# Two feed-forward layers on one core: 96 in place of 128 weight columns in one of five output products

## The chip, the cores and the metric

The kernel runs on one core of one Trainium2 chip. A core has five engines that run side by side and meet at semaphores: TensorE (PE, the matrix multiplier, whose weight loads the profile lists apart as PEld), VectorE (DVE), ScalarE (ACT), GpSimd (POOL) and SyncE (SP, which here only issues DMAs). The metric is the time of one execution on the device in microseconds; the median of several runs counts.

## The reference, cut to what matters

A softmax-weighted causal convolution of seven taps over 8192 tokens of 192 features, then two feed-forward layers:

```python
gate = 1.0 / (1.0 + np.exp(-(x @ w_gate)))        # x (8192, 192), w_gate and w_val (192, 1536)
y = gate * (x @ w_val) @ w_out                    # w_out (1536, 192)
h = y @ w_in                                      # w_in (192, 2048)
g = np.where(h > 0.0, h, np.exp(np.minimum(h, 0.0)) - 1.0)
z = g @ w_out2                                    # w_out2 (2048, 192)
```

Everything is float32.

## The kernel before

Features and hidden units lie on the partitions, tokens along the free axis. The tokens are cut into 16 blocks of T = 512. For each block there is a G phase (the gated layer: 12 tiles of 128 hidden units) and an E phase (the second layer: 16 tiles of 128, taken in 8 pairs).

Each float32 operand of a matmul is split into a high part and a low part (what the rounding of the high part left over), both of type fp32r. A product is then made of high by high, low by high and high by low. Low by low is not wanted: it is smaller than the rest by the square of the rounding.

TensorE works in two halves. A matmul on `rows` LOW (partitions 0 to 63) and one on UP (64 to 127) run side by side, each with its own weights of 64 rows by 128 columns, and each streams the 512 tokens. The code interleaves the two: in the loop over `s`, one LOW and one UP matmul are issued in turn. I call such a pair of places a slot. A G step (one tile) has 14 slots: 9 for the hidden units (`hid_mm`, HID = 9) and 5 for a tile's share of the outputs (`product`). LOW takes its 9 hidden matmuls first and the 5 products after, UP the 5 products first. An E step (a pair of tiles) has 19 slots, 9 and 10.

The 192 outputs of a layer lie in two banks. `acc[0]` (`y_acc_a`, `z_acc_a`) holds the first 128 outputs. `acc[1]` (`y_acc_b`, `z_acc_b`) holds the last 64 twice over: its lower 64 partitions sum the products with the high part of the weights, its upper 64 those with the low part, and the two halves are added later (ACT's `take_y_b` or `take_z`, then DVE). The weights for this lie side by side in 128 columns that begin at `both_b`: 64 high columns, then 64 low columns. The five kinds of `product` are:

- 0: high part of the hidden tile by the high weights of the first 128 outputs
- 1: low part of the hidden tile by the same weights
- 2: high part by the low weights of the first 128 outputs
- 3: high part by the 128 columns at `both_b`
- 4: low part by the 128 columns at `both_b`

So in kind 4 the first 64 columns give a wanted sum (low by high), and the last 64 give low by low. A matmul of kind 4 also carries semaphore increments: `share_done` on LOW, `up_b_done` on UP at the end of a step's products.

The last four tiles of the whole run have no partner. Their 20 products run after the last slot on all 128 rows at once. Over the run there are 5100 slots with two matmuls and 20 with one, 10220 matmuls in all, each with a weight load of its own.

Around this ACT bends (`curve`) and makes the high parts, DVE multiplies, makes the low parts and sums the taps, SP issues the loads of weights and tokens and the stores.

Of the kernel before, what the change touches and what calls it, by code (L numbers as in the profile page):

```python
# [12 lines left out]
P = 128  # L13
# [3 lines left out]
MAIN = 3 * P + OUT  # L17
LOW = slice(0, HALF)
UP = slice(HALF, P)
HID = 9  # L20
RING = 4
RAW_G_SLOTS = 8
# [11 lines left out]
def ffn_kernel(nc, conv_w, x_windows, g_weights, e_weights, out):  # L34
# [16 lines left out]
    with ExitStack() as ctx:  # L51
# [114 lines left out]
        def _(sp):  # L166
# [15 lines left out]
            def swap_x(j):  # L182
                sp.wait_ge(x_ready, 2 * j + 1)
                sp.dma_start(xs[LOW, 4:6].bitcast(F32), xs[UP, 0:2].bitcast(F32)).then_inc(x_swapped, 16)
                sp.dma_start(xs[UP, 4:6].bitcast(F32), xs[LOW, 0:2].bitcast(F32)).then_inc(x_swapped, 16)

            def swap_y(n, inp=ys):
                sp.wait_ge(y_free, 2 * n + 1)
                sp.dma_start(inp[LOW, 4:6].bitcast(F32), inp[UP, 0:2].bitcast(F32)).then_inc(y_swapped, 16)
                sp.dma_start(inp[UP, 4:6].bitcast(F32), inp[LOW, 0:2].bitcast(F32)).then_inc(y_swapped, 16)  # L190

# [39 lines left out]
        def _(pe):  # L231
            def hid_mm(rows, acc, w, inp, s, last=HID - 1):


                part, kind = divmod(s, 3)
                at = P * part + (MAIN + HALF if kind == 2 else 0)
                features = (0, 4, 2)[part] + (1 if kind == 1 else 0)
                return nc.tensor.matmul(acc[:], w[rows, at:at + P], inp[rows, features],  # L238
                                        start=s == 0, stop=s == last)
# [6 lines left out]
            def e_tile_share(t, base, acc):  # L246
                at, lo_a = (3 * P, 3 * P + MAIN + HALF) if t % 2 == 0 else (2 * MAIN, 2 * MAIN + 2 * P)
                return Share(acc, ew[:, t // 2], at, at + P, lo_a, t % RING, base + t + 1,
                             t == 0, t == NE - 1)

            def product(rows, share, kind, start, stop):


                at = (share.hi_a, share.hi_a, share.lo_a, share.both_b, share.both_b)[kind]
                part = (0, 1, 0, 0, 1)[kind]
                return nc.tensor.matmul(share.acc[kind // 3][:], share.w[rows, at:at + P],  # L256
                                        h_split[rows, share.slot, part], start=start, stop=stop)

            def share_and_kind(shares, k):


                tiles = len(shares)
                if k < 2 * tiles:
                    return shares[k // 2], 2 * (k % 2)
                if k < 3 * tiles:
                    return shares[k - 2 * tiles], 1
                return shares[(k - 3 * tiles) // 2], 3 + (k - 3 * tiles) % 2
# [4 lines left out]
            def up_share_waits(shares, k, step):  # L272
                share, kind = share_and_kind(shares, k)
                if kind == 0:
                    pe.wait_ge(hi_done, share.done)
                if kind == 1:
                    pe.wait_ge(lo_done, share.done)
                if k == 0:
                    wait(pe, low_a_done, step - LAG)
                if k == 3 * len(shares):  # L280
                    wait(pe, share_done, shares[0].done - 1)

            def low_share_waits(shares, k, step):
                if k == 0:
                    pe.wait_ge(up_a_done, step - LAG + 1)
                if k == 3 * len(shares):
                    pe.wait_ge(up_b_done, step - LAG + 1)

            def up_share(shares, k):
                share, kind = share_and_kind(shares, k)  # L290
                mm = product(UP, share, kind, share.first and kind in (0, 3), False)
                if k == 3 * len(shares) - 1:
                    mm.then_inc(up_a_done, 1)
                if k == 5 * len(shares) - 1:
                    mm.then_inc(up_b_done, 1)

            def low_share(shares, k):
                share, kind = share_and_kind(shares, k)
                mm = product(LOW, share, kind, False, share.last and kind in (1, 4))
                if k == 3 * len(shares) - 1:  # L300
                    mm.then_inc(low_a_done, 1)
                if kind == 4:
                    mm.then_inc(share_done, 1)

            def opening(inp):


                def both(t, part, kind):
# [3 lines left out]
                    lower = hid_mm(LOW, gate, gw[:, t], inp, s, last)  # L312
                    upper = hid_mm(UP, val, gw[:, t], inp, s, last)
                    if s == last:
# [32 lines left out]
            def g_phase(base, step, n, prev, inp=xs, acc=y_acc):  # L347
# [9 lines left out]
                for t in range(0 if prev else 3, NG):  # L357
# [18 lines left out]
                    count = 5 * len(shares)  # L376
                    for s in range(HID + count):
                        if s < count:
                            up_share_waits(shares, s, step + t)
                        if s >= HID:  # L380
                            low_share_waits(shares, s - HID, step + t)
                        if s == count and prev == "E" and t < 2:
                            pe.wait_ge(hidden_done, base - 2 + 2 * t)
                        if s < HID:
                            mm = hid_mm(LOW, gate, gw[:, t], inp, s)
                            if s == HID - 1:
                                mm.then_inc(hid_done, 1)
# [61 lines left out]
            for t in range(NE - 4, NE - 1):  # L449
                share = e_tile_share(t, end + NE, y_acc)  # L450
                pe.wait_ge(hi_done, share.done)
                product(slice(0, P), share, 0, False, False)
                product(slice(0, P), share, 2, False, False)
                product(slice(0, P), share, 3, False, False)
                pe.wait_ge(lo_done, share.done)
                product(slice(0, P), share, 1, False, False)
                product(slice(0, P), share, 4, False, False).then_inc(share_done, 1)
            share = e_tile_share(NE - 1, end + NE, y_acc)
# [445 lines left out]
```

## Time and profile before

| | us |
|---|---|
| median of 3 runs | 1187.38 (1187.08 to 1187.71) |
| the profiled execution, its time | 1185.75 |
| the profiled execution, its span | 1184.0 |
| TensorE matmul busy in the span | 1166.5 (99%) |
| TensorE weight load busy | 1058.8 (89%) |
| VectorE busy | 925.2 (78%) |
| ScalarE busy | 629.8 (53%) |
| GpSimd busy | 89.6 (8%) |

The page of the profile gives each engine's busy time, then the span in 40 slices, the DMA queues, the chain of work that ended last, and the costliest groups of instructions. Matmuls are pipelined and their ends are modelled. The start times in the timeline are therefore the ones to read, and a duration of 386 ns for a matmul doesn't mean that the next one starts 386 ns later. The span begins with the first instruction; the run's time is 1.75 us longer than it. The granted TensorE clock over the span is 1.000 of full speed.

### The profile page before, as it was taken

The numbers are of one execution on the slowest core, as the hardware profiler recorded it, in microseconds if no ns is written. First come the engines' busy times: TensorE is split into PE (matmuls) and PEld (weight loads), VectorE is DVE, ScalarE is ACT, GpSimd is POOL, SyncE is SP. The second block draws the span as 40 slices with busy tenths as digits, with TensorE's granted clock in tenths as the row PEclk, the third lists the DMA queues.
The fourth block names the chain that finished last, engine by engine and source line by source line (L and its number), as shares of the span: only waits on it lengthen the run. The fifth ranks groups of instructions, "written<-read, shape, count | busy, mean of one in ns | idle before, by whom it ended". The sixth has DMA issues, their size and how long they took to land.

```text
span 1184.0 us, 27136 instructions
## 1 busy us (share of the span) xinstructions
PE 1166.5 (99%) x10220; PEld 1058.8 (89%) x10220; DVE 925.2 (78%) x1497; ACT 629.8 (53%) x1093; POOL 89.6 (8%) x87
## 2 busy tenths in 40 slices
PE   5999999999999999999999999999999999999998
PEld 4988889998888888888888899999999889999998
DVE  7888777787777877778777787777777777787786
ACT  6556545465554555545455464554646545465554
POOL 4371001010010100101000010100101001010000
PEclk9999999999999999999999999999999999999999
DMA  6021101001010010100101001110101101001000
GB/s 209 20 72 37 32 18 35 31 18 31 18 35 31 18 31 18 42 25 18 31 18 49 18 18 31 36 31 18 24 24 36 31 18 35 31 18 31 10 11 27
DMA packets 14022, 38.04 MB, mean 32 GB/s; under 512 B 2224, under 2 KB 2224, under 8 KB 14000
## 3 DMA queue, kind: packets, MB, share of 16 engines
q1 hardware_dynamic: 13776, 37.60, 10.9%
q8 instruction: 15, 0.25, 0.1%
q10 hardware_dynamic: 224, 0.14, 0.1%
q14 instruction: 7, 0.06, 0.0%
HBM read 15.71 MB, written 6.29 MB: 19 GB/s over the span
## 4 chain that ended last, share of the span: by engine, by line
PE 97%; POOL 1%; DVE 1%; DMA 1%; ACT 0%; issue 0%; SPq 0%; DVEq 0%
PE hid L238 54%; PE z_acc_a L256 15%; PE y_acc_a L256 11%; PE z_acc_b L256 9%; PE y_acc_b L256 7%; POOL gw L815 1%; DMA raw_g<-g_weights 1%; DVE mixed L648 0%; POOL gw L823 0%; PE y_acc_a L238 0%; DVE ys L655 0%; SPq L175 0%; PE y_acc_b L238 0%; ACT ys L606 0%; DVE z_out L702 0%
## 5 line engine op out<-in xcount | busy, mean ns | idle before, releaser
L238 PE MATMUL hid<-xs,gw 64*128 64x512 f32 x3240 | 606.0, 386 | 0.0
L238 PEld LDWEIGHTS hid<-xs,gw 64*128 64x128 f32 x3240 | 501.7, 184 | 35.6 <-DVE h_split L675 0.6
L238 PE MATMUL hid<-ys,ew 64*128 64x512 f32 x2160 | 478.5, 387 | 0.0
L489 ACT CAST h_split<-hidden 128x512 fp32r<-128x512 f32 x448 | 277.0, 618 | 273.2 <-DVE hidden L717 231.4
L484 ACT ACTIVATE curve<-hid 128x512 f32<-128x512 f32 x446 | 263.3, 597 | 262.5 <-PE hid L238 262.3
L238 PEld LDWEIGHTS hid<-ys,ew 64*128 64x128 f32 x2160 | 376.2, 184 | 25.4 <-DVE h_split L675 0.8
L256 PE MATMUL z_acc_a<-h_split,ew 64*128 64x512 f32 x1440 | 365.4, 387 | 0.0
L675 DVE TENSOR_TENSOR h_split<-hidden,h_split 128x512 fp32r<-128x512 f32 x448 | 318.2, 710 | 32.7 <-ACT h_split L489 27.4
L256 PE MATMUL y_acc_a<-h_split,gw 64*128 64x512 f32 x1080 | 302.7, 386 | 0.0
L256 PEld LDWEIGHTS z_acc_a<-h_split,ew 64*128 64x128 f32 x1440 | 264.6, 184 | 15.1
L256 PE MATMUL z_acc_b<-h_split,ew 64*128 64x512 f32 x960 | 256.2, 386 | 0.0
L717 DVE TENSOR_TENSOR hidden<-hid,curve 128x512 f32<-128x512 f32 x190 | 131.3, 691 | 132.7 <-PE hid L238 109.4
L256 PE MATMUL y_acc_b<-h_split,gw 64*128 64x512 f32 x720 | 220.7, 386 | 0.0
L256 PEld LDWEIGHTS y_acc_a<-h_split,gw 64*128 64x128 f32 x1080 | 196.0, 184 | 8.3
L256 PEld LDWEIGHTS z_acc_b<-h_split,ew 64*128 64x128 f32 x960 | 176.7, 184 | 9.8
L751 DVE SCALAR_TENSOR_TENSOR hidden<-hid,below 128x512 f32<-128x512 f32 x256 | 177.1, 692 | 8.8
L748 DVE TENSOR_SCALAR below<-curve 128x512 f32<-128x512 f32 x256 | 114.9, 449 | 72.4 <-ACT curve L484 71.9
L633 DVE SCALAR_TENSOR_TENSOR mixed<-x_in,taps,mixed 128x512 f32<-128x512 f32 x192 | 147.3, 767 | 0.0
L256 PEld LDWEIGHTS y_acc_b<-h_split,gw 64*128 64x128 f32 x720 | 132.5, 184 | 6.4
L803 POOL TENSOR_TENSOR xs<-mixed,xs 128x512 fp32r<-128x512 f32 x14 | 25.7, 1835 | 926.1 <-ACT xs L493 926.1
L238 PE MATMUL hid<-ys,gw 64*128 64x512 f32 x180 | 32.7, 408 | 13.8 <-ACT ys L601 11.4
L528 ACT ACT_TABLE_LOAD x31 | 39.8, 1283 | 1.7 <-PEq L897 1.2
(74 smaller groups left out, 465.3 us busy)
## 6 DMA issues: line engine op xcount, KB each, us to landing
x_in<-x_windows SPq DMA_DIRECT2D x16, 518.0 KB, 3.2
ys<-ys SPq DMA_DIRECT2D x30, 256.0 KB, 3.6
xs<-xs SPq DMA_DIRECT2D x30, 256.0 KB, 3.4
out<-z_out SPq DMA_DIRECT2D x16, 256.0 KB, 2.0
raw_g<-g_weights SPq DMA_DIRECT2D x12, 288.0 KB, 5.8
raw_e<-e_weights SPq DMA_DIRECT2D x8, 384.0 KB, 4.0
out<-z_out SPq DMA_DIRECT2D x15, 128.0 KB, 2.3
x_in<-x_windows SPq DMA_DIRECT2D x2, 259.0 KB, 4.1
```

Source lines behind the costliest of these rows:

```text
L238: return nc.tensor.matmul(acc[:], w[rows, at:at + P], inp[rows, features], start=s == 0, stop=s == last)
L256: return nc.tensor.matmul(share.acc[kind // 3][:], share.w[rows, at:at + P], h_split[rows, share.slot, part], start=start, stop=stop)
L484: nc.scalar.activation(curve[:, t % 2], source[:], func).then_inc(curve_done, 1)
L489: nc.scalar.copy(h_split[:, t % RING, 0], hidden[:, t % RING]).then_inc(hi_done, 1)
L528: nc.scalar.activation(warm[:], warm[:], func).then_inc(table_set, 1)
L633: mix = nc.vector.scalar_tensor_tensor(mixed[:, c], token, taps[:, c, k:k + 1], mixed[:, c], ALU.mult, ALU.add)
L675: nc.vector.tensor_tensor(h_split[:, t % RING, 1], hidden[:, t % RING], h_split[:, t % RING, 0].bitcast(F32), ALU.subtract).then_inc(lo_do ...
L717: nc.vector.tensor_tensor(hidden[:, t % RING], val[:], curve[:, t % 2], ALU.mult).then_inc(hidden_done, 1)
L748: nc.vector.tensor_scalar(below[:, t % 2], curve[:, t % 2], 1.0, -1.0, ALU.min, ALU.add).then_inc(below_done, 1)
L751: nc.vector.scalar_tensor_tensor(hidden[:, t % RING], hid[t % 4][:], 0.0, below[:, t % 2], ALU.max, ALU.add).then_inc(hidden_done, 1)
L803: nc.gpsimd.tensor_tensor(xs[:, 1], mixed[:, 0], xs[:, 0].bitcast(F32), ALU.subtract).then_inc(x_ready, 1)
L815: nc.gpsimd.tensor_tensor(tile[:, MAIN + HALF:2 * MAIN], raw[:, 0:rest], tile[:, 0:rest].bitcast(F32), ALU.subtract).then_inc(g_ready, 1)
```

## The change

A constant `FEW = 96` is added. In `product` a matmul of kind 4 that doesn't close its accumulation takes 96 columns of weights in place of 128 and writes 96 partitions of `acc[1]` in place of 128. The columns left out are the last 32 of the 64 that give low by low. The matmul that closes an accumulation (`stop`) keeps 128 columns.

```diff
+FEW = 96
...
                 part = (0, 1, 0, 0, 1)[kind]
-                return nc.tensor.matmul(share.acc[kind // 3][:], share.w[rows, at:at + P],
+                cols = FEW if kind == 4 and not stop else P
+                return nc.tensor.matmul(share.acc[kind // 3][0:cols], share.w[rows, at:at + cols],
                                         h_split[rows, share.slot, part], start=start, stop=stop)
```

The number of instructions, their order, their waits and what they stream (512 tokens) stay as they were. Of the 10220 weight loads 860 become narrower: 444 on UP, 413 on LOW and 3 of those on all 128 rows.

## Rows read from the trace of the kernel before

**Rows 1.** The page: busy time of each engine, share, number of instructions.

```profile
PE 1166.5 (99%) x10220; PEld 1058.8 (89%) x10220; DVE 925.2 (78%) x1497; ACT 629.8 (53%) x1093; POOL 89.6 (8%) x87
```

**Rows 2.** Waits of PE: who waited for whom, us in total, times, longest.

```profile
PE hid L238 <- ACT ys L601: 11.4, 1, 11.4
PE hid L238 <- ACT ys L606: 1.1, 1, 1.1
PE hid L238 <- POOL gw L823: 0.6, 1, 0.6
PE hid L238 <- DVE h_split L675: 0.4, 1, 0.4
PE hid L238 <- issue: 0.2, 1, 0.2
```

**Rows 3.** Timeline of PE, first and last of twelve G steps: start, us, instructions.

```profile
569.21 0.39 PE L256 MATMUL y_acc_b<-h_split,gw 64*128 64x512 f32 x1
569.22 1.51 PE L238 MATMUL hid<-xs,gw 64*128 64x512 f32 x10
...
604.12 1.51 PE L238 MATMUL hid<-ys,ew 64*128 64x512 f32 x10
```

**Rows 4.** Timeline of PE, then of PEld, around 606 us.

```profile
605.93 0.39 PE L238 MATMUL hid<-ys,ew 64*128 64x512 f32 x1
605.94 0.39 PE L256 MATMUL y_acc_b<-h_split,gw 64*128 64x512 f32 x1
606.15 0.39 PE L238 MATMUL hid<-ys,ew 64*128 64x512 f32 x1
606.16 0.39 PE L256 MATMUL y_acc_b<-h_split,gw 64*128 64x512 f32 x1
606.38 0.39 PE L256 MATMUL z_acc_a<-h_split,ew 64*128 64x512 f32 x1
606.39 0.39 PE L238 MATMUL hid<-ys,ew 64*128 64x512 f32 x1
...
605.93 0.18 PEld L238 LDWEIGHTS hid<-ys,ew 64*128 64x128 f32 x1
605.94 0.18 PEld L256 LDWEIGHTS y_acc_b<-h_split,gw 64*128 64x128 f32 x1
606.22 0.18 PEld L238 LDWEIGHTS hid<-ys,ew 64*128 64x128 f32 x1
606.25 0.32 PEld L256 LDWEIGHTS z_acc_a<-h_split,ew 64*128 64x128 f32 x2
```

**Rows 5.** Timeline of PE, then of PEld, after a stop of PE in the opening.

```profile
23.79 0.50 PE L238 MATMUL hid<-ys,gw 64*128 64x512 f32 x1 [0.40 <-DVE h_split L675]
24.13 0.39 PE L238 MATMUL hid<-ys,gw 64*128 64x512 f32 x1
...
23.79 0.18 PEld L238 LDWEIGHTS hid<-ys,gw 64*128 64x128 f32 x1 [0.83 <-DVE h_split L675]
23.80 0.18 PEld L256 LDWEIGHTS z_acc_a<-h_split,gw 64*128 64x128 f32 x1
23.90 0.19 PEld L238 LDWEIGHTS hid<-ys,gw 64*128 64x128 f32 x1
```

**Rows 6.** Timeline of PE at the end: last half-row matmuls, then the full-row products.

```profile
1175.10 0.39 PE L238 MATMUL hid<-xs,ew 64*128 64x512 f32 x1
1175.51 0.70 PE L256 MATMUL y_acc_a<-h_split,ew 128*128 128x512 f32 x2
1176.04 0.39 PE L256 MATMUL y_acc_b<-h_split,ew 128*128 128x512 f32 x1
...
1178.76 0.84 PE L256 MATMUL y_acc_b<-h_split,ew 128*128 128x512 f32 x3
1179.44 0.84 PE L256 MATMUL y_acc_a<-h_split,ew 128*128 128x512 f32 x3
```

**Rows 7.** The page's groups: matmul and load of one bank of kinds 3 and 4.

```profile
L256 PE MATMUL z_acc_b<-h_split,ew 64*128 64x512 f32 x960 | 256.2, 386 | 0.0
L256 PEld LDWEIGHTS z_acc_b<-h_split,ew 64*128 64x128 f32 x960 | 176.7, 184 | 9.8
```

## The prediction

> **What bounds the kernel now.** I read the page first, for the engine with no air: TensorE is busy for 1166.5 us of 1184.0, VectorE for 925.2, ScalarE for 629.8 [rows 1]. Then the waits of PE: they come to 13.7 us, all at line 238, each of them seen once, and 11.4 of it is the start of the run, before the first input is there [rows 2]. From the opening on nothing ever holds TensorE up, so the time is the number of slots times the length of one, plus a start and an end.
>
> The length of a slot comes out of the timeline by start times. The same place of a G step (the run of ten hidden matmuls) begins at 569.22 and, eleven steps of 14 slots later, at 604.12 [rows 3]: 34.90 us / 154 = 226.6 ns. All 5120 slots at that make 1160.2 us. The remaining 23.8 us of the span of 1184.0 are the 13.7 us of waits, slower first slots, and the evacuation and store after the last matmul. A slot streams 512 columns, at the full clock of 2.4 GHz (granted 1.000 over the span) 213.3 ns. So 13.3 ns of each slot are not the stream, and this surplus is the only part of a slot that a narrower load can shorten; the moving data is as long as before.
>
> **Whether the load sets the pace.** Three views bear on it. First, the load's own time where nothing covers it: after a stop, loads for both halves begin at 23.79 and 23.80, the next load of the first half at 23.90, and the second matmul at 24.13. The stopped matmul is shown at 0.50 us where others take 0.39 [rows 5]. Both say 0.11 us for a load of 128 columns, and the two halves load at the same time. Second, a load that begins late. As a rule a load starts with the matmul before it. At 606 us it doesn't: the loads begin at 606.22 and 606.25, and their matmuls start at 606.39 and 606.38, which are 0.24 and 0.22 us after their forerunners at 606.15 and 606.16 [rows 4]. A load begun 0.13 us ahead of its matmul is therefore early enough, while the usual head start is 0.226 us. A load has about 0.1 us to spare. Third, the end of the run, where a slot has one load for all 128 rows and not two: from 1176.04 to 1178.76 are twelve slots, 226.7 ns each [rows 6]. Two loads per slot or one makes no difference. Nothing here lets the duration of a load enter the slot as such.
>
> **The change part by part.** The 860 narrower loads: 444 tiles have paired products (448 less the last four), so 444 on UP. On LOW the last tile of each phase closes its sum and stays at 128: 31 such phases outside the tail, 413 left. The tail has 3. If a load's uncovered time goes with its columns, each falls from 0.11 to 0.08 us, 0.03 us x 860 = 26 us of loading less. All of it lies under matmuls, with 0.1 us of cover, and is worth nothing by itself. Were that cover gone, what is late next is the stream, 13.3 ns away.
>
> How many slots could be shortened at all? LOW and UP start within 0.01 us of each other [rows 4], in turn. The UP matmul of kind 4 comes early in a step and its LOW neighbour is a full-width hidden matmul; the LOW one comes late beside a full-width UP. A shorter place on one half lets that half slip ahead within the slot but not past the other. Over a step each half has one shorter place per tile, and the gain of a step is one such place per tile, not two. So 413 + 3 = 416 slots count.
>
> The price of 32 columns within the surplus isn't in any row, since every load has 128. Bounds: at one end 0, the surplus belongs to the start of a matmul or the change of weights, however many columns. At the other end the whole 13.3 ns, as if 96 columns no longer met whatever 128 do: 416 x 13.3 = 5.5 us. Between them, in proportion: 13.3 x 32/128 = 3.3 ns, 416 x 3.3 = 1.4 us. I take 0. The nearest row is the slot of the tail: half as many loads, the same 226.7 ns. The late loads point the same way: they overlap their stream at another place, and the slot stays within the 0.01 us that the timeline resolves.
>
> The Trainium skill speaks against that choice. "TensorE: Matmul & The Clock Gate", section "Back-to-back issue gap", gives 215.7 ns as the isolated spacing at 512 columns and says that with a load for each matmul the spacing is set by both operations. Its section "LDWEIGHTS (loading the stationary operand)" has a load take columns / 1.2 ns: 107 ns for 128 and 80 ns for 96, an estimate of 27 ns less. The first figure agrees with the 0.11 us of [rows 5]. By these two, were the load in the way, the 27 ns would be cut off at the surplus, the end of 5.5 us above. The same page's "What happens when you issue a matmul" gives loads a read port of their own, by which the gain would be 0.
>
> Fewer written partitions: a matmul of kind 4 writes 96 partitions per column in place of 128. In the rows all kinds, b banks and hidden banks alike, take the same slot, and writing keeps up with the stream. 0. The increments `share_done` and `up_b_done` ride on matmuls of kind 4. ACT waits for the first, but has 554 us of idle time [rows 1], and PE's own waits on the second are never seen [rows 2]. 0. DVE and ACT read `acc[1]` over all its partitions as before. 0.
>
> Sum: 0 on the profiled 1185.75. That run lies 1.6 us under the median of 1187.38, and against the median the forecast is 1187.4.
>
> **The rivals.**
>
> *In proportion.* The surplus is a collision of loading and streaming, say, so many reads of each. 1.4 us less, 1186.0. For it: loads overlap every stream. Against it: the tail. It can't be told from no change.
>
> *The surplus goes.* Up to 5.5 us, 1181.9. It needs 5.8 ns or more of the 13.3 per changed slot to be over 0.2% (2.4 us / 416). For it: the surplus exists, and no matmul in the trace is without a load, so nothing shows that it isn't the load's. Against it: the 0.1 us of slack.
>
> *Slower: a load of another width isn't drawn ahead.* The engine fills the next weights while a matmul runs. It may do so only when the shape of both is the same. Such a load would lie open, 0.11 us as in [rows 5] for each of 860: 95 us, 1282. From 2.8 ns per changed load (2.4 us / 860) this decides the sign. For it: the one change of shape in the trace, from half rows to full rows, isn't smooth. The last half-row matmul starts at 1175.10, the first full-row one at 1175.51 with its pair 0.70 us long, the third at 1176.04 [rows 6]. Counted back two slots from 1176.04 the first began in effect at 1175.59, 0.26 us after the half-row stream could have been followed. If each narrow matmul changed the mode of the array twice, 860 x 2 x 0.26 = 447 us, 1635. Against it: that row changes the number of rows, while the change leaves the rows as they are and still takes more than half of the columns. In the Trainium skill "TensorEngine Tiling (Array Packing)", "Key Properties", says that a change of tiling mode drains the engine, which the gap at 1175 agrees with. "PSUM — Partial Sum Buffer", "The four PSUM rules", says that float32r matmuls force the column group to the whole width, by which 96 columns would be no change of mode; no row here shows that.
>
> *The change doesn't do what it says.* The load may still fetch 128 columns in the hardware, or the 32 columns may be loaded as nothing. Time 1187.4.
>
> **How the numbers follow.** No change 0.60, in proportion 0.16, not done 0.04: together 0.80 within 0.2%, which is about what a measurement of this kernel can tell from no change. The surplus goes, wholly or by more than 5.8 ns: 0.10. Slower by loads that lie open or a drain: 0.10, of which 0.02 is the drain. The likeliest is 1187.4. The range goes down to the full surplus, 1181.9 less the 0.3 us by which the runs differ, 1181.6. Upward it goes by the 1.6 us that lie between the profiled run and the median, 1189.0. That holds all but the slower cases, 0.9; the cap of the unknown price asks for the lower end.
>
> **What the profile of after would show.** Narrow loads in groups of their own, with a mean under the 184 ns of [rows 7]. If no change is right: the eleven G steps still take 34.90 us, PE idle still only in the opening, PEld's busy time some 10 to 25 us lower than 1058.8. In proportion: 34.86. If the surplus goes: 34.75, one slot in 14 at 213 ns. If loads lie open: matmuls of 0.50 us at line 256 in every step, and a step of 3.39 us or more in place of 3.17. I would be wrong on the main step if a slot with a narrow load starts its successor earlier than 226.6 ns by more than 5 ns, or later by more than 3.

## The result and the profile after

The changed kernel takes 1195.06 us (median of 4 runs, 1195.01 to 1195.49), beside 1187.23 for the kernel before in the same comparison. The ratio is 1.0066, with a 95% interval of 1.0053 to 1.0079. I had forecast 1187.4 and at most 1189.0. Nothing was gained, and 7.8 us were lost with less data loaded.

The page of the profiled execution (span 1193.7 us, 9.7 more than before; its time 1195.49) gives this line for the busy times, the counterpart of [rows 1]:

```profile
PE 1177.7 (99%) x10220; PEld 1138.0 (95%) x10220; DVE 925.1 (78%) x1497; ACT 630.2 (53%) x1093; POOL 89.7 (8%) x87
```

VectorE, ScalarE and GpSimd are busy as long as before. TensorE has 11 us more. PEld rises by 79 us, although 860 loads are shorter. These figures are unions over the two halves: where both load at the same moment the time counts once. Before, the halves mostly started close together; now they are apart. UP started its place of a slot 17 ns after LOW in the median before (never more than 111), and 143 ns in the median after, at times 356.

The waits of PE, as in [rows 2], have not grown:

```profile
PE hid L239 <- ACT ys L604: 10.8, 1, 10.8
PE hid L239 <- POOL gw L826: 0.5, 1, 0.5
PE hid L239 <- DVE h_split L678: 0.4, 1, 0.4
PE hid L239 <- ACT ys L609: 0.4, 1, 0.4
```

The groups of PEld with shapes kept apart show that the change does what it says, and what a narrow load takes (rows as in [rows 7]; the last figures are the busy time, the mean ns of one and the idle time ahead):

```profile
L259 PEld LDWEIGHTS z_acc_b<-h_split,ew 64*128 64x128 f32 x495 | 91.2, 184 | 0.1
L259 PEld LDWEIGHTS z_acc_b<-h_split,ew 64*96 64x96 f32 x465 | 73.4, 158 | 0.1
L259 PEld LDWEIGHTS y_acc_b<-h_split,gw 64*128 64x128 f32 x375 | 69.1, 184 | 1.9
L259 PEld LDWEIGHTS y_acc_b<-h_split,gw 64*96 64x96 f32 x345 | 54.4, 158 | 1.9
```

26 ns less for 32 columns. The whole loss is in the length of the slots, as the timeline of PE shows over one G step. The same place of the step, the first product of the UP half:

```profile
572.42 0.39 PE L259 MATMUL y_acc_a<-h_split,gw 64*128 64x512 f32 x1
...
575.64 0.39 PE L259 MATMUL y_acc_a<-h_split,gw 64*128 64x512 f32 x1
```

3.22 us in place of the 3.173 of [rows 3].

To see more than the two decimals of the timeline, I took the start of each matmul from the trace in whole ns. A slot below is the time from one matmul of a half to the next of the same half. "Excess" is the sum over one half of each slot less the even length (226 2/3 ns, 226.7 for short), from 41 us on, as a mean of the two halves.

| slots of both halves | before: number, mean ns | after: number, mean ns | excess before, us | excess after, us |
|---|---|---|---|---|
| in which the next load is narrow | - | 847, 230.0 | - | 1.4 |
| in which the running matmul is narrow | - | 846, 232.1 | - | 2.3 |
| that touch nothing narrow | 9986, 227.1 | 8289, 228.7 | 2.1 | 8.6 |
| all | 9986, 227.1 | 9982, 229.1 | 2.1 | 12.3 |

10.2 us more per half, 0.6 us less at the start of the run: the 9.7 us of the span. Of the 10.2 only 3.7 are in slots with a narrow load or matmul. The rest is in slots whose instructions are what they were. That was the question for the experiments.

### The profile page after: what moved, and what is told of

It is laid out like the page before. It is cut to its first block, busy times and chain, and to the rows that moved or that the text cites. A ratio compares the mean times of both kernels' runs of the same rounds, so it can differ in the third digit from the quotient of the medians.

```text
span 1193.7 us, 27136 instructions
## 1 busy us (share of the span) xinstructions
PE 1177.7 (99%) x10220; PEld 1138.0 (95%) x10220; DVE 925.1 (78%) x1497; ACT 630.2 (53%) x1093; POOL 89.7 (8%) x87
## 3 DMA queue, kind: packets, MB, share of 16 engines
q1 hardware_dynamic: 13776, 37.60, 10.9%
## 4 chain that ended last, share of the span: by engine, by line
PE 97%; POOL 1%; DVE 1%; DMA 0%; ACT 0%; issue 0%; SPq 0%; DVEq 0%
PE hid L239 55%; PE z_acc_a L259 13%; PE y_acc_a L259 11%; PE z_acc_b L259 9%; PE y_acc_b L259 8%; POOL gw L818 1%; DMA raw_g<-g_weights 0%; DVE mixed L651 0%; POOL gw L826 0%; PE y_acc_a L239 0%; ACT L531 0%; SPq L176 0%; DVE ys L658 0%; ACT ys L609 0%; DVE z_out L705 0%
## 5 line engine op out<-in xcount | busy, mean ns | idle before, releaser
L239 PE MATMUL hid<-xs,gw 64*128 64x512 f32 x3240 | 612.2, 389 | 0.0
L239 PEld LDWEIGHTS hid<-xs,gw 64*128 64x128 f32 x3240 | 509.9, 184 | 15.4
L239 PEld LDWEIGHTS hid<-ys,ew 64*128 64x128 f32 x2160 | 369.4, 184 | 6.6
L678 DVE TENSOR_TENSOR h_split<-hidden,h_split 128x512 fp32r<-128x512 f32 x448 | 318.2, 710 | 32.6 <-ACT h_split L492 27.4
L259 PE MATMUL z_acc_b<-h_split,ew 64*128 64x512 f32 x960 | 259.8, 389 | 0.0
L259 PE MATMUL y_acc_b<-h_split,gw 64*128 64x512 f32 x720 | 223.7, 390 | 0.0
L259 PEld LDWEIGHTS y_acc_a<-h_split,gw 64*128 64x128 f32 x1080 | 199.1, 184 | 3.5
L259 PEld LDWEIGHTS z_acc_b<-h_split,ew 64*128 64x128 f32 x960 | 164.6, 171 | 0.2
L259 PEld LDWEIGHTS y_acc_b<-h_split,gw 64*128 64x128 f32 x720 | 123.6, 172 | 3.8
L239 PE MATMUL hid<-ys,gw 64*128 64x512 f32 x180 | 33.4, 417 | 12.3 <-ACT ys L604 10.8
L239 PEld LDWEIGHTS hid<-ys,gw 64*128 64x128 f32 x180 | 24.8, 200 | 17.3 <-ACT ys L604 10.8
```

The source lines that it names most:

```text
L259: return nc.tensor.matmul(share.acc[kind // 3][0:cols], share.w[rows, at:at + cols], h_split[rows, share.slot, part], start=start, stop=stop)
L678: nc.vector.tensor_tensor(h_split[:, t % RING, 1], hidden[:, t % RING], h_split[:, t % RING, 0].bitcast(F32), ALU.subtract).then_inc(lo_do ...
```

## The experiments

Each kernel was timed beside the kernel before on its chip. The kernel before was not at the same time everywhere: its median was 1187.2 in the first comparison, 1184.9, 1188.5, 1184.6, 1188.5 and 1187.5 in the others. "Over before" is against the median of its own comparison. The last column is the excess of one half in the trace, which doesn't depend on that median. For the kernel before it comes from the one execution that was traced, of 1185.75 us. `w64` (1189.91) and `up_quarter` (1189.11) lie within 1.5 us of the kernel before's highest median, so that for these two the excess is the safer figure.

| kernel | odd matmuls | us | ratio to before, 95% interval | over before, us | excess, us |
|---|---|---|---|---|---|
| before | 0 | - | - | - | 2.1 |
| the change | 860 narrow | 1195.06 | 1.0066 (1.0053 to 1.0079) | 7.8 | 12.3 |
| up_only | 444 narrow | 1194.90 | 1.0084 (1.0068 to 1.0101) | 10.0 | 12.2 |
| low_only | 413 narrow | 1195.33 | 1.0088 (1.0071 to 1.0105) | 10.4 | 12.3 |
| w112 | 860 of 112 columns | 1192.25 | 1.0062 (1.0045 to 1.0079) | 7.3 | 9.6 |
| w64 | 860 of 64 columns | 1189.91 | 1.0042 (1.0026 to 1.0059) | 5.0 | 7.4 |
| w120 | 860 of 120 columns | 1194.40 | 1.0083 (1.0066 to 1.0099) | 9.8 | 11.3 |
| quarter | 223 narrow | 1191.55 | 1.0027 (1.0016 to 1.0037) | 3.1 | 7.4 |
| up_quarter | 111 narrow | 1189.11 | 1.0038 (1.0024 to 1.0053) | 4.5 | 6.4 |
| half | 446 narrow | 1195.49 | 1.0091 (1.0074 to 1.0108) | 10.9 | 12.6 |
| kinds34 | 1720 narrow | 1195.59 | 1.0060 (1.0043 to 1.0077) | 7.1 | 12.8 |
| inner96 | 8812 narrow | 1203.89 | 1.0129 (1.0112 to 1.0146) | 15.4 | 21.6 |
| tok480 | 860 of 480 tokens | 1191.22 | 1.0025 (1.0015 to 1.0034) | 2.7 | 8.5 |
| tok504 | 860 of 504 tokens | 1198.20 | 1.0115 (1.0098 to 1.0132) | 13.6 | 15.3 |
| all96 | all of 96 columns | 1201.48 | 1.0109 (1.0092 to 1.0126) | 13.0 | 17.5 |
| all112 | all of 112 columns | 1211.69 | 1.0218 (1.0191 to 1.0244) | 24.2 | 27.4 |
| all504 | all of 504 tokens | 1184.16 | 0.9963 (0.9949 to 0.9977) | -4.3 | 2.2 |
| all480 | all of 480 tokens | 1146.13 | 0.9651 (0.9635 to 0.9668) | -41.4 | -35.5 |
| again | 860 narrow | 1195.16 | 1.0055 (1.0039 to 1.0072) | 6.7 | 12.3 |

**One half alone.** `up_only` and `low_only` narrow kind 4 on one half:

```diff
-                cols = FEW if kind == 4 and not stop else P
+                cols = FEW if kind == 4 and rows == UP else P
```

> Only the UP half's products of kind 4 are 96 wide (444), LOW stays at 128. In the trace of the changed kernel a slot in which a narrow load or a narrow matmul takes part is about 230 ns instead of 226.7, so each narrow product costs its own half 2 x 3.4 = 6.7 ns; the kernel as changed has 860 of them and is 7.8 us slower, of which 413 x 6.7 = 2.8 us is one half's own. Theory A, own cost alone: the UP half needs 444 x 6.7 = 3.0 us more and holds LOW back by the order of issue: 1190.2 us. Theory B, most of the loss comes from the two halves disturbing each other (slots of 231 to 236 ns that touch no narrow load): with one half undisturbed much less than half of the 7.8 us is lost if both must be narrow, about 1189; or about half or more, 1191 to 1193, if one half's narrow loads are enough to lengthen the other half's slots. Rival C, a fixed cost per narrow load whatever the half: 444/860 x 7.8 = 4.0 us, 1191.2.

> Only the LOW half's products of kind 4 are 96 wide (413, not the tail's). Theory A (own cost alone, 6.7 ns each): 2.8 us, 1190.0 us. Theory B (the halves disturb each other): as for UP alone, 1189 if both must be narrow, 1191 to 1193 if one is enough. Rival C (a fixed cost for each): 413/860 x 7.8 = 3.7 us, 1190.9. UP alone and LOW alone together should come to the whole 7.8 us under C, to less than it if the halves' losses only partly hide each other, and clearly less under B with both needed.

Half of the narrow loads, on either half, cost as much as all of them (1194.90 and 1195.33 against 1195.06 and 1195.16). Theory A and rival C as priced fall: they gave 1190.0 to 1191.2. What of B is right the places in a step show. These are the ns over 226.7 of each place of a G step, place 0 to 13, in the mean of 149 steps of `up_only`, where UP's narrow matmul is at place 4:

```
UP    0.1  0.0  0.1  3.3  3.3  8.3  6.6  9.2 -2.5  4.2  9.2  1.6  5.8  4.2   sum 53
LOW  15.8  5.5  9.1  0.4  4.0  4.7  1.1  2.1  1.8  0.0  0.2 -0.2  0.2  1.6   sum 46
```

UP loses 3.3 ns while the narrow load is under way and 3.3 while the narrow matmul runs, as in the change. Then it loses 46 ns more over nine places at which everything is 128 wide. LOW has nothing narrow at all. It loses 16 ns in the slot of place 0, where the code has the step's waits for the hidden tiles and shares that come out of both halves, and 30 ns in the uneven slots behind it. So the price of a narrow matmul in a G step is 53 ns on its half, and the other half is held back by nearly as much. It isn't held back at once: in 91 of the 127 steps of 19 slots, in each of which UP loses its 20 ns, LOW runs even and UP falls behind. That the two halves meet again later, and that in the change both lose time side by side, is why two halves cost no more than one. The sum for UP goes up: 188 steps with one narrow matmul x 53 ns, and 128 steps of 19 slots with two, which lose 20 ns each (places 6 to 10: 3.3, 3.4, 3.4, 5.8, 4.2), are 12.5 us, beside the 12.3 that were measured in all.

**Other widths.** `w112`, `w64` and, later, `w120` change one number:

```diff
-FEW = 96
+FEW = 112
```

> As changed, but 112 columns in place of 96. If the cost lies in the change of width from one load to the next, whatever the width, this is as slow as 96 columns: 1195.0 us. If it goes with the number of columns left out, half of the loss: 1191.1. If it has to do with a 32-column strip of the array that is left out altogether, 112 columns still touch all four strips and the time is that of the kernel before, 1187.3.

> As changed, but 64 columns in place of 96, which is all that is wanted of the product. If the cost is that of any change of width: 1195.0 us. If it goes with the columns left out: twice the loss, 1202.8. If 64 columns put the array in another mode that must drain on the way in and out (0.26 us as at the end of the run of before, at most 2 x 860 times): up to 447 us more, 1634. If a still shorter load gained something against the 13.3 ns of surplus in a slot, under 1195.

> As changed, with 120 columns: 8 columns less in place of 32. Theory D (any departure of a slot from 226.7 ns sets off a train, whatever its size): about the loss of 112 and 96 columns, 6 to 10 us over the kernel before. If the cost goes with the columns left out: a quarter of 7.8 us, 2 us. If it needs a strip of 32 left out: 0.

Eight columns fewer cost more than 64 fewer (9.8 and 5.0 us over before, 11.3 and 7.4 us of excess). The loss doesn't grow with the columns left out, nor does it need a strip of 32 columns left out, which also rules out a change of the array's mode: 447 us were never near. What is left out matters for the slots that touch the narrow load (226.8 ns in the mean when the next load has 64 columns, 232.5 when it has 120), and not in an order that I can explain.

**How often.** The same figures stand in single steps, to the ns, and in the kernel before as well. Here is UP around its narrow matmul at 583.0 us in `up_quarter`, then UP in the changed kernel from 592.5 us on, then LOW in the kernel before, after a stop of PE at 66.2 us (from one start to the next; the bars mark the train):

```
up_quarter, UP:           226 227 | 230 230 235 233 236 224 231 236 228 233 231 | 226 227
the change, UP:           226 227 | 230 230 235 233 236 224 231 236 228 233 231 | 226 227
before, LOW:      227 227 238 335 | 235 233 236 224 231 236 228 233 231 | 226 227
```

A disturbed half doesn't return to 226.7 ns at once. It runs through a fixed train of uneven slots and is even again only behind it. The train of eleven slots is 53 ns longer than eleven even ones, a short one of its last five (231 236 228 233 231) 26 ns. The kernel before pays for trains too, and not only behind a stop of PE. Of its excess of 2.1 us, 1.4 us on LOW and 1.1 us on UP lie in two steps of each block, the third and fourth of the E phase. In none of these is a slot longer than 285 ns, and in many none is longer than those of a train. One of the many begins right behind the late loads of [rows 4]. UP's starts there, after the 606.38 of those rows:

```profile
606.61 0.39 PE L256 MATMUL z_acc_a<-h_split,ew 64*128 64x512 f32 x1
607.08 0.39 PE L256 MATMUL z_acc_a<-h_split,ew 64*128 64x512 f32 x1
607.78 0.39 PE L256 MATMUL z_acc_b<-h_split,ew 64*128 64x512 f32 x1
```

From 606.38 to 607.78 are six slots, 233 ns each. In ns they are 226 231 238 233 235 233, and a 230 follows: 39 ns more than even. Whether the late loads set them off isn't shown.

`quarter` has one narrow tile in four, `up_quarter` (`and rows == UP`) the same on UP alone, `half` (`share.slot % 2 == 0`) one tile in two:

```diff
+                cols = FEW if kind == 4 and share.slot == 0 and not stop else P
```

> 96 columns only in every fourth tile (t = 0, 4, 8, 12): 223 narrow loads in place of 860. So far UP alone, LOW alone and both were each about 10 us over the kernel before on their chip, or 8 to 10, so the loss doesn't add up. In the traces a narrow load is followed by a train of uneven slots that touch no narrow load (231, 236, 228, 233, 231 ns, then 226.7 again; or 235, 233, 236, 224 ahead of these), and the same train stands in the kernel before behind every wait of PE. Theory D (a disturbance sets off a train of 5 to 9 slots that costs 25 to 47 ns, and trains that overlap don't add): 111 disturbances on each half, 25 to 47 ns each, 3 to 5 us per half: 4 to 6 us over the kernel before, more than the quarter of the loss. Rival C (a cost for each narrow load, whatever its neighbours): 223/860 of 8 to 10 us, 2.0 to 2.6 us over.

> 96 columns on the UP half alone, in every fourth tile: 111 narrow loads, about four steps apart. Theory D (trains): each narrow load sets off one train on UP of some 53 ns, read from the run with a quarter of the tiles (230, 230, 235, 233, 236, 224, 231, 236, 228, 232, 231 against 226.7). If trains stay on their half, LOW's slots stay at 226.7 and UP needs 111 x 0.053 = 5.9 us more, of which the order of issue passes on all to the end: about 3 us as in the quarter run or up to 5.9 us over the kernel before. If a train also sets off one on the other half, LOW shows 235 ns slots of its own without any narrow load. Rival C (each narrow load for itself): 111/860 of 8 to 10 us, 1.0 to 1.3 us.

> 96 columns in every second tile on both halves: 446 narrow loads. A quarter (223) gave 3.1 us, all (860) 7.8, all of one half (444 or 413) 10.0 and 10.4, each against the kernel before on its chip. Theory D with trains that overlap: between the quarter and the whole, 5 to 9 us. Rival C: 446/860 x 7.8 = 4.0 us.

The excess goes from 2.1 (none) to 6.4 (111 on UP), 7.4 (223), 12.6 (446) and 12.3 (860). A quarter of the narrow loads brings half of the excess, a half of them all of it. A narrow load costs most where it stands alone. In an E step of the change, two stand at places 7 and 9 and cost 20 ns together; in `half`, where only one of the two is left, it sets off the long train, and the E step loses 52 ns (UP, places 6 to 16: 3.5 3.5 8.1 6.4 8.7 -2.3 3.9 8.7 1.6 5.5 3.9). In `quarter` and in `up_quarter` alike 111 trains of 53 ns are 5.9 us on a half. 5.3 and 4.3 were measured (7.4 and 6.4, less 2.1). In `up_quarter` LOW lost as much as UP (excess 6.3 and 6.5) with no narrow load of its own, so the loss does pass to the other half whole.

It passes late and in trains. Through the 19-slot steps from 543 to 569 us of `up_quarter` LOW runs even, while UP's lag behind it grows from 30 to 190 ns, by 53 with each narrow load. From 575 us on LOW begins each G step with a short train (231 236 228 233 231), also in steps in which UP is even and so catches up by 27 ns. Of the 137 steps of 14 slots without a narrow load on UP, LOW loses more than 20 ns in 112. So it isn't only waiting: much of LOW's loss is in trains of its own, which begin where a step begins. Neither outcome that I had listed for LOW is quite this one.

**The rhythm disturbed without a narrow load.** The decisive pair. All loads have 128 columns, and kind 4 streams fewer tokens, that is, TensorE has less to do:

```diff
+                few = 480 if kind == 4 and not stop else T
+                return nc.tensor.matmul(share.acc[kind // 3][:, 0:few], share.w[rows, at:at + P],
+                                        h_split[rows, share.slot, part, 0:few], start=start, stop=stop)
```

> All loads at 128 columns, but kind 4 streams 480 of the 512 tokens (the low by high product is left out for the last 32 tokens of a block). It is a disturbance of the rhythm without a narrow load, and with less work: 32 columns less at 2.4 GHz is 13.3 ns, over 416 slots of one half 5.5 us less. Theory D: shorter matmuls set off the same trains as narrow loads (231, 236, 228, 233, 231 ns), which cost 25 ns and more and eat the 13.3 ns: no faster than the kernel before, rather 2 to 6 us slower. Rival (the cost belongs to the width of the load): 5.5 us faster than before, all other slots at 226.7.

> All loads at 128, kind 4 streams 504 tokens in place of 512 (low by high is left out for the last 8 tokens of a block): 8 columns or 3.3 ns less, the size of what a narrow load adds to its slot, with the other sign. By the stream alone 416 x 3.3 = 1.4 us faster than before. Theory D (a departure of 3 ns either way sets off a train): slower than before, by 4 to 9 us, with slots of 231 to 236 ns behind each kind 4. If small departures heal at once and only the 13.3 ns of 480 tokens or a narrow load do it: 0 to 1.4 us faster.

Both are slower than the kernel before, the smaller cut by far. In `tok504` the same place of two G steps, again from the timeline of PE:

```profile
595.61 0.38 PE L259 MATMUL y_acc_b<-h_split,gw 64*128 64x504 f32 x1
...
598.83 0.38 PE L259 MATMUL y_acc_b<-h_split,gw 64*128 64x504 f32 x1
```

3.22 us once more, though the step has less to stream. In ns the short matmul's slot on UP is 223, as 8 columns less at 2.4 GHz would have it, and behind it stand 234 231 233 236 224 231 236 228 233 231. The 3.3 ns won cost 50 ns. All told a G step of UP is 47 ns longer than even and an E step 53, where in E steps the narrow loads had only 20 ns; this is why `tok504` loses more than the change. With 480 tokens the slot is 214 (13 ns won), and all told a G step of UP is 36 ns longer and an E step 16. Theory D's main claim is shown: a slot that is 3 ns shorter, with all loads at 128, sets off the same train as a narrow load, with one uneven slot more. The rival, a cost that belongs to the width of the load, gave 5.5 us faster and falls. The size of the train isn't explained by the size of the kick: with 64 columns the place of the narrow matmul and the three after it lose 8.7, 1.7, 5.7 and 4.0 ns and no more, 20 in all, which is why `w64` is the mildest of the widths.

**More of the same width.** Kinds 3 and 4 narrow, then everything but the matmuls that open or close a sum:

```diff
-                cols = FEW if kind == 4 and not stop else P
+                cols = FEW if kind in (3, 4) and not (start or stop) else P
```

> Kinds 3 and 4 both take 96 columns (the low weights of the last 32 outputs are left out of the result): some 1690 narrow loads, but kinds 3 and 4 follow each other on a half, so that the width changes at 2 places in a step and half, where the changed kernel has 2 in a G step and 4 in an E step. Cost for each narrow load: twice the loss, 16 to 20 us over the kernel before. Cost for each change of width: fewer changes in E, the same in G, about three quarters of the loss, 6 to 8 us. Theory D (each change is a disturbance that sets off a train): as by changes, 6 to 8 us; slots between two narrow loads are 226.7 ns or shorter, not 230.

> Every matmul takes 96 columns but those that open or close an accumulation (upper 32 outputs of each are incomplete, so most of the result is wrong in them): 7 of 9 hidden matmuls and nearly all products, over 8500 narrow loads, with runs of 5, 7 or 10 of them. It asks whether the 13.3 ns by which a slot exceeds its stream is the load's. If it is: slots inside the runs of 216 ns or less, and the kernel up to 40 us faster than before. If the surplus is fixed: 226.7 inside the runs. Cost for each narrow load: ten times the loss, 80 us slower. Cost for each change of width (about 4 in a step and half): 8 to 14 us slower.

`kinds34` gives the loss of the change for twice the narrow loads: not by load. But theory D expected even slots of 226.7 between two narrow loads, and they are not even: 230.4 ns in the mean of 1071 slots in `kinds34`, and again in the 7314 slots of `inner96`. The even rhythm did not come back where neighbours were alike. So either narrow loads are slow as such (rival E below), or the runs of them were too short.

**Everything alike.** All matmuls of the run get the same shape, with the rest of the banks set to zero at the start. This is `all96`; `all112` has 112 columns, and `all504` and `all480` keep 128 columns and cut the tokens to 504 or 480:

```diff
-                cols = FEW if kind == 4 and not stop else P
+                cols = FEW
...
-                return nc.tensor.matmul(acc[:], w[rows, at:at + P], inp[rows, features],
+                return nc.tensor.matmul(acc[0:FEW], w[rows, at:at + FEW], inp[rows, features],
...
+            for bank_ in (*hid, *y_acc, *z_acc):
+                nc.vector.memset(bank_[FEW:P], 0.0)
```

> Every matmul of the run takes 96 columns (the upper 32 outputs of each are left out and stand at zero, so a quarter of each hidden tile is missing from the result; VectorE writes the zeros first, which delays the opening by some 1 to 4 us). All slots are alike again. Theory D (what costs is that a slot differs from its neighbours): slots of 226.7 ns without trains, and the time of the kernel before plus that delay, 1185 to 1192. If the 13.3 ns of surplus is the load's in proportion to its columns: 223.3 ns, 17 us less. If all of it: 213 to 216 ns, 55 to 68 us less. Rival E (a narrow load as such costs, and only 128 columns run evenly): slots of 230 ns and more everywhere, as in the runs of 96-wide matmuls of the run before (mean 230.4), 1200 to 1206.

> Every matmul takes 112 columns. With 96 everywhere the slots were 228 to 232 ns, 230.2 in the mean, and the run 13 us slower than the kernel before, so narrow loads that are all alike are slower than 128-wide ones too. If that goes with the columns left out: 228.4 ns, 1194. If any width under 128 loses the even rhythm of 226.7: about 230 again, 1201. If it takes a strip of 32 columns left out: 226.7, 1187 to 1190.

> Every matmul streams 504 tokens in place of 512, all loads at 128 (the last 8 tokens of each block are left out). Only kind 4 at 504 tokens was 13.6 us slower than the kernel before. Theory D (unequal slots set off trains, equal ones don't): slots of 226.7 - 3.3 = 223.3 ns, no trains, 5120 x 3.3 = 17 us faster than the kernel before. Rival F (the even rhythm hangs on the length of 512 itself): uneven slots throughout, around 230, 10 to 20 us slower than before.

> Every matmul streams 480 tokens (the last 32 of each block are left out), all loads at 128. With 504 tokens everywhere the slots stayed at 226.7 ns, though the stream is 3.3 ns shorter, so a slot isn't the stream plus a fixed surplus. If something other than the stream paces it (the loads, or an instruction's own path): 226.7 ns again, the time of all504, 1184. If a slot is the stream rounded up to a step of 13.3 ns (512 and 504 tokens land on the same one): 213.3 ns, 5120 x 13.3 = 68 us less than all504, 1116. If stream plus 13.3 holds after all and 504 was a chance: 213.3 too; if a half step: 220.

The timeline of PE in `all96`, then `all504`, then `all480`, the same half in each:

```profile
597.03 0.39 PE L239 MATMUL hid<-xs,gw 64*96 64x512 f32 x1
...
597.72 0.39 PE L239 MATMUL hid<-xs,gw 64*96 64x512 f32 x1
```

```profile
586.66 0.39 PE L259 MATMUL y_acc_a<-h_split,gw 64*128 64x504 f32 x1
...
587.34 0.39 PE L259 MATMUL y_acc_b<-h_split,gw 64*128 64x504 f32 x1
```

```profile
566.84 0.37 PE L259 MATMUL y_acc_a<-h_split,gw 64*128 64x480 f32 x1
...
567.48 0.38 PE L259 MATMUL y_acc_b<-h_split,gw 64*128 64x480 f32 x1
```

Each pair is three slots apart: 0.230, 0.227 and 0.213 us a slot. In ns, with the means over the whole run from 41 us on:

| kernel | columns, tokens | typical slots, ns | mean slot, ns |
|---|---|---|---|
| before | 128, 512 | 226 227 227, even | 227.1 |
| all504 | 128, 504 | 226 227 227, even | 227.1 |
| all480 | 128, 480 | 212 221 212 221, or 215 to 218 | 219.6 |
| all96 | 96, 512 | 232 228 230 230, never even | 230.2 |
| all112 | 112, 512 | 233 234 233 on one half, 225 to 232 on the other | 232.2 |

Two things fall here. With 8 tokens less in every matmul the slot is as long as before, so a slot is not its stream plus a fixed surplus. And with 16 or 32 columns less in every load it is longer, so the width is not hidden from it. `all96` says which of the two it was: narrow loads that are all alike are slower too, which is rival E, and theory D's "equal slots don't cost" holds for 128 columns only. `all504` answers rival F (the rhythm hangs on the length of 512) halfway: the even rhythm doesn't hang on 512 tokens, but its slot didn't shorten to 223.3 as theory D had it. 4.3 us of gain against before are near the 4 us by which the kernel before itself differs from comparison to comparison. `all480` came out at none of the lengths that I had listed. In `all96` the halves run 20 ns apart and PEld is busy for 912.5 us, and the slots are long nonetheless, so the distance between the halves isn't the cause; nor is it in the kernel before, where slots are 226.9 ns in the mean at 15 to 30 ns of distance and 227.0 at 80 to 100 ns.

**Once more.**

> The changed kernel once more, on the chip and beside the runs of before that the two others are compared with. The kernels with trains in every step gave 1194.9 to 1195.6 on four chips' runs, the kernel before 1184.6 to 1188.5. Theory D: 1195 again, 7 to 10 us over the kernel before, by what the kernel before happens to give.

1195.16 beside 1188.48. The change lies at 1195 both times; what moves is the kernel before.

What stays open is why. 128 columns with 512 or 504 tokens run evenly, slot after slot. The other pairs that ran throughout (96 or 112 columns with 512 tokens, 128 columns with 480) have uneven slots. A half that has lost the rhythm takes 4 to 11 slots to find it again. The runs show this and its size. They don't part the load from its matmul: each narrow load is followed by a matmul that uses 96 columns and writes 96 partitions, so when I speak of the load's width, it is the width of the pair. Which part of the engine or of the memory is behind it they don't show, and I leave it at that. A kernel with 64 columns in every load was not run. No variant that computes the whole result beat the kernel before.

## Why the prediction was wrong

- **What bounds the kernel** held: TensorE without a stop behind the opening, and the time is slots times their length. So did the start, the count of 860, and the busy times of all other engines. (The last row of [rows 3] is an E step; the first two E steps of a block have 14 slots too, so the 226.6 ns stand.)
- **The 13.3 ns surplus** was the first step that failed. I took the slot as 213.3 ns of stream plus 13.3 of something, from one pair of lengths. `all504` has 210 ns of stream and the same 226.7.
- **"The load is covered"** was the step on which the forecast rested. The uncovered time was rightly sized: 0.03 us less was the estimate from [rows 5], 26 ns the measurement. The three views still prove less than I drew from them. The late loads at 606 us [rows 4] show that a load may begin 0.1 us late and its own matmul still be in time. Half by half both matmuls come 0.23 us after their forerunners (my 0.24 and 0.22 mixed the halves). But I stopped reading there: the seven slots of UP behind them are 39 ns longer than even, in the view that I took for slack. The full-row slots of [rows 6] show that one load or two is the same. Both have loads of 128 columns, and neither says that a load of another width leaves the slot alone. My text said that the price "isn't in any row, since every load has 128", and then bounded it between 0 and a gain: I let the cover fix the sign of the unknown. The price was a loss: 3.3 ns in the slot that loads it and 5.4 in the one that runs it (230.0 and 232.1 less 226.7), and then the trains. The 3.3 ns are just past the 3 that I had named as the sign of being wrong on this step.
- **416 slots, not 860** was argued from an order of issue by which a half can't slip past the other. The halves of the changed kernel are up to 356 ns apart, more than a slot. That one half's loss counts once was right, for another reason: they work side by side and meet again at the waits between steps, after up to 0.36 us apart.
- **"Zero" for the matmuls that don't change** was the largest miss: 6.5 of the 10.2 us of a half. I summed the price of changed instructions and took the others as fixed. That a PE stream has a memory could have been seen ahead. The trace of the kernel before has the trains behind its stops, and in the 23.8 us that 5120 even slots left of the span I passed over the 2.1 that lie in uneven slots behind the opening.
- **The slower rival** had the right sign and the wrong mechanism. It put the load in the open, 0.11 us each and 1282 us. Groups of 0.50 us did not appear. I had set 2.8 ns per changed load as the point from which it decides; the measured loss is 7.8 us / 860 = 9.1 ns each. A chance of 0.10 for everything above 1189 was too low for an operation with no row of its own.
- **The gain rivals** ("in proportion", "the surplus goes") fell with `all96`: of its 9990 slots from 41 us on only 3 are under 228 ns.
- **The pages.** The Trainium skill, "TensorE: Matmul & The Clock Gate", section "LDWEIGHTS (loading the stationary operand)", gives, as an estimate by its columns / 1.2 ns, 27 ns less for 32 columns; the trace agrees with 26 (184 to 158). Its "What happens when you issue a matmul" says that the load has a read port of its own and takes no read bandwidth from the running matmul. From that I drew a gain of 0. No run tests the port; but the same stream with narrower loads took 230.2 ns in place of 226.7, so the width does enter the slot, and what I drew was wrong. "Back-to-back issue gap" says that both operations set the spacing; in that it was nearer than my reading, though not in the sign that I drew from it. (The 215.7 ns stand under another heading of the page; this section has about 216.) "TensorEngine Tiling (Array Packing)", "Key Properties", on the drain between modes: no such drain was seen (a narrow matmul that stands alone costs its half some 53 ns, not 0.26 us), nor need there have been one by what "PSUM — Partial Sum Buffer" says of float32r.

## What to carry to other kernels

- Where TensorE runs without a gap at one even slot length, that evenness is worth something, and a matmul or load of another shape in it can cost more than it saves. Here 3.3 ns less work cost 50 ns. Price such an edit as a disturbance of 20 to 53 ns each on its half, times how many can run out before the next, and don't treat "less work under cover" as zero at worst.
- Before trusting a cover argument for a resource, ask whether any row shows that resource at another size; if none does, the range must go to both sides.
- Measure start to start in ns around the few stops that a steady kernel has: how it settles again shows what any odd instruction will cost.

## What the runs showed of the hardware that I had not expected

- A paired slot of 64-row matmuls at the full clock is 226.7 ns with 128-column loads and 504 or 512 tokens, 219.6 in the mean with 480 tokens, 230.2 with 96-column and 232.2 with 112-column loads and 512 tokens.
- After a stop or an odd matmul a half runs through the same train each time: 231 236 228 233 231 ns, often with 235 233 236 224 ahead of it. The other half, with other rows, weights and banks, doesn't take it over at once: in `up_quarter` it ran even until it was 0.19 us ahead, and then lost the same in short trains at the start of its steps.
- A load of 96 columns is recorded at 158 ns against 184 for 128, and the kernel is slower for it.
- The kernel before moves by 4 us between comparisons (medians of 1184.6 to 1188.5), and within two of them (1184.5 to 1188.2, 1184.5 to 1189.0), while `up_only`, `low_only`, `half`, `kinds34` and the change itself stay within 1194.9 to 1195.6. Whether its own trains account for that was not tested.
